# An expert-tile loop on the vector engine that begins at another instruction of the same sequence

## What is computed

```python
logits = xn @ en.T / tau
expert_idx = np.argmax(logits, axis=1)
...
for e in range(E):                      # E = 8 experts
    mask = expert_idx == e
    if not mask.any():
        continue
    h = np.maximum(x[mask] @ w1[e], 0.0)             # 512 -> 1024
    out[mask] = gate_w[mask, None] * (h @ w2[e])     # 1024 -> 512
```

## Time and profile before

| | us |
|---|---|
| median of 3 runs | 1535.5 (1533.52 to 1538.3) |
| the profiled execution's own time | 1540.79 |
| its span, first to last instruction | 1539.0 |
| TensorE busy in the span | 1442.9 (94%) |
| VectorE busy in the span | 920.7 (60%) |

### The profile page before, as it was taken

One profiled execution on the slowest core, in us unless ns is written; L12 is line 12 of the kernel. 1 busy time (PEld: TensorE's weight loads), 2 busy tenths in 40 slices (PEclk: granted clock), 3 DMA queues, 4 the chain that ended last, 5 costly groups with the idle time before them and its releaser, 6 DMA issues.

```text
span 1539.0 us, 27343 instructions
## 1 busy us (share of the span) xinstructions
PE 1442.9 (94%) x8080; PEld 1226.6 (80%) x8081; DVE 920.7 (60%) x1784; ACT 768.3 (50%) x1559; POOL 397.7 (26%) x348
## 2 busy tenths in 40 slices
PE   4799999999999999999999999999999899899996
PEld 3678888888888888888888888877888778678785
DVE  7886677878577878667887766675314123232221
ACT  3666666675657666656666566652323123132220
POOL 3433233334233343324333323231000000000000
PEclk9899999999999999999999999998999999999999
DMA  9532012212001221101121002025312211311110
GB/s 193 148 94 79 1 45 47 64 36 53 9 25 44 47 68 34 37 1 52 42 65 40 22 1 76 1 97 193 116 44 90 94 42 53 131 34 47 41 39 25
DMA packets 139524, 91.18 MB, mean 59 GB/s; under 512 B 118873, under 2 KB 119129, under 8 KB 139233
## 3 DMA queue, kind: packets, MB, share of 16 engines
q1 hardware_dynamic: 132784, 70.12, 17.1%
q0 software_dynamic: 5840, 18.92, 3.3%
q10 hardware_dynamic: 736, 0.29, 0.1%
HBM read 70.39 MB, written 21.28 MB: 60 GB/s over the span
## 4 chain that ended last, share of the span: by engine, by line
PE 56%; DVE 22%; issue 10%; ACT 6%; POOL 3%; DMA 1%; DVEq 1%; ACTq 1%; SPq 0%; POOLq 0%
PE ps L530 17%; PE ps L531 17%; PE ps L532 17%; DVE gs L1003 5%; DVE gs L1000 2%; DVE kfold L1029 2%; ACT gs L804 2%; DVE gs L1008 2%; PE ps L713 2%; DVE k_sb L1035 2%; DVE qrec L1022 1%; POOL g_lo L1397 1%; DVE ps L1001 1%; ACT q_sb L831 1%; PE ps L685 1%
## 5 line engine op out<-in xcount | busy, mean ns | idle before, releaser
L1397 POOL TENSOR_TENSOR g_lo<-gs,g_hi 128x384 fp32r<-128x384 f32 x192 | 205.3, 1069 | 420.2 <-ACT g_hi L809 419.0
L530 PE MATMUL ps<-x_hi,wi_hi 128*128 128x384 f32 x768 | 277.0, 361 | 0.8 <-issue 0.8
L531 PE MATMUL ps<-x_lo,wi_hi 128*128 128x384 f32 x768 | 261.4, 340 | 0.0
L532 PE MATMUL ps<-x_hi,wi_lo 128*128 128x384 f32 x768 | 261.2, 340 | 0.0
L530 PE MATMUL ps<-wo_hi,g_hi 128*128 128x512 f32 x576 | 233.1, 405 | 26.5 <-POOL g_lo L1397 26.2
L531 PE MATMUL ps<-wo_lo,g_hi 128*128 128x512 f32 x576 | 231.0, 401 | 0.0
L532 PE MATMUL ps<-wo_hi,g_lo 128*128 128x512 f32 x576 | 229.6, 399 | 0.0
L799 ACT ACTIVATE usq<-ps 128x384 f32<-128x384 f32 x192 | 93.8, 488 | 250.8 <-PE ps L532 250.8
L920 ACT ACTIVATE hb<-ps 128x512 f32<-128x512 f32 x74 | 44.3, 598 | 330.9 <-PE ps L532 330.9
L1000 DVE SCALAR_TENSOR_TENSOR gs<-gs,ps 128x384 f32<-128x384 f32 x192 | 106.0, 552 | 169.0 <-ACT gs L804 167.5
L1003 DVE TENSOR_TENSOR gs<-gs,usq 128x384 f32<-128x384 f32 x192 | 175.4, 914 | 0.0
(11 more groups left out here) (209 smaller groups left out, 2698.8 us busy)
## 6 DMA issues: line engine op xcount, KB each, us to landing
w_raw<-w SPq DMA_DIRECT2D x10, 2048.0 KB, 9.0
xrow<-scratch SPq DMA_DIRECT2D x37, 257.0 KB, 2.7
q_sb<-q SPq DMA_DIRECT2D x62, 144.0 KB, 3.0
k_sb<-k SPq DMA_DIRECT2D x62, 144.0 KB, 3.1
v_sb<-v SPq DMA_DIRECT2D x60, 144.0 KB, 3.3
in_raw<-w_in SPq DMA_DIRECT2D x8, 512.0 KB, 5.9
out_raw<-w_out SPq DMA_DIRECT2D x8, 512.0 KB, 5.6
scratch<-pad_d SPq DMA_DIRECT2D x8, 257.0 KB, 4.5
```

Of the source, the lines that this page charges most:

```text
L530: mm(out_, a_hi, b_hi, start=first, stop=False)
L531: mm(out_, a_hi, b_lo, start=False, stop=False)
L532: return mm(out_, a_lo, b_hi, start=False, stop=last)
L1397: G.tensor_tensor(g_lo[:, (s - 1) % 3], gs[:, (s - 1) % 2], g_hi[:, (s - 1) % 3].bitcast(F32), ALU.subtract).then_inc(glo_ready, 1)
```

## The change

The body that was `slot` (splits, then scaling) is cut in two. `splits(t)` is all of a tile but the scaling. The loop's turn now begins with `scaled(4i)` and ends with `splits(4i + 4)`; `splits(4)` is written out ahead of the loop and `scaled(32)` behind it. The sequence of vector work that is executed stays the same, instruction for instruction: what moves is the place in it at which the branch back is taken. The other four engines' programs are as before.

```diff
-        def slot(t, j, ahead1, ahead2, stored):
-            with live(dve, t):
-                if ahead1:
-
-                    weights(t, T_SOLE, range(4))
-                h_split(t, j)
-                if ahead2:
-                    with live(dve, t + 2):
-                        t_split(t + 2, (j + 2) % 4)
-                if ahead1:
-                    weights(t, T_NEW, (0, 1))
-                    weights(t, T_SECOND, (2, 3))
-                scaled(t, j, stored)
+        def splits(t, j, ahead1, ahead2):
+
+            if ahead1:
+                weights(t, T_SOLE, range(4))
+            h_split(t, j)
+            if ahead2:
+                with live(dve, t + 2):
+                    t_split(t + 2, (j + 2) % 4)
+            if ahead1:
+                weights(t, T_NEW, (0, 1))
+                weights(t, T_SECOND, (2, 3))
...
-        slot(3, 3, True, True, None)
+        splits(3, 3, True, True)
+        scaled(3, 3, None)
+        splits(4, 0, True, True)
         with dve.Fori(1, LOOPS) as i:
             for j in range(4):
-                slot(i * 4 + j, j, True, True, i * 16)
-        for t in range(4 * LOOPS, TILES):
-            slot(t, t % 4, t + 1 < TILES, t + 2 < TILES, 16 * (t // 4))
+                scaled(i * 4 + j, j, i * 16)
+                splits(i * 4 + (j + 1), (j + 1) % 4, True, True)
+        scaled(4 * LOOPS, 0, 16 * LOOPS)
+        for t in range(4 * LOOPS + 1, TILES):
+            with live(dve, t):
+                splits(t, t % 4, t + 1 < TILES, t + 2 < TILES)
+                scaled(t, t % 4, 16 * (t // 4))
```

## The result

| | before | changed |
|---|---|---|
| median | 1534.5 us (1533.0 to 1538.3, 4 runs) | 1514.3 us (1512.5 to 1516.1, 4 runs) |
| span of the profiled execution | 1539.0 us | 1510.6 us |
| granted clock, mean | 0.981 | 0.988 |

The ratio is 0.9864, with a 95% interval of 0.9842 to 0.9887: 20 us faster, between 17 and 24. The forecast was 1512.1 us, 23.4 us faster.

A forecast was written before the change was run, and what follows sets the result against it. TensorE was taken to bound the kernel, stalled by VectorE's late h_lo at six branches back. Idle 15.6 us plus 7.8 us of slower matmuls make 23.4; 1535.5 - 23.4 = 1512.1 us, range 1508.5 to 1519.

The forecast's parts named there:

- What bounds the kernel: Expert tiles: TensorE, 94% busy, waits 18.3 us for VectorE's h_lo, late behind six branches back; 15.6 us idle there.
- The pauses are the fetch of code: At VectorE's branch back, pauses of 2.87 and 1.94 us were taken for fetching code not on the engine.
- the second question of the prediction: Whether VectorE's pauses go away or are only covered; expected gone, the sum hardly depending on it.
- The three pieces against four: VectorE's old loop body was placed in four 8 KB code pieces, the new one in three, so pauses should go.
- The rival that the stall is not the branch's: Stall belongs to table reading or what follows tile 4i + 3, staying before h_lo; no change, 1535.5 us; chance 0.06.
- The cover and the slack: Moved branch back has 5.4 us of idle cover before osb; osb may then be 4.2 us late at no cost.
- the turn of tile 24: VectorE also writes weights there, so less cover: 0.3 us cost for one pause, 2.2 us idle for both.
- slower: Rival: pause outgrows cover, slack and old loss, above 13.5 us a turn; at 16 us a turn, 1550 us; chance 0.03.
- The size: Gain of 23.4 us: all six stretches holding a branch back fall to 12.50 us, 15.6 idle plus 7.8 slower matmuls.

The follow-up runs named there:

- a_fill71: Changed kernel with 71 never-executed instructions ahead of the loop, so it begins, modulo 128, where the loop of before begins; 1515.7 us, ratio 0.9890.
- a_again10: Changed kernel with the first scaling of each loop turn made 10 times more, so osb comes late; 1561.8 us, ratio 1.0176.
- b_same: Kernel before, unchanged, run once more for a second profile; its six stretches lost 19.6 us.
- b_fill128: Kernel before with 128 never-executed instructions in tile 3's skipped T_SOLE body, ahead of the loop; 1534.0 us, ratio 0.9997.
- a_long128: Changed kernel with 128 never-executed instructions inside the loop, in the skipped T_SOLE body of tiles 4i + 1; 1516.6 us, ratio 0.9886.
- a_again4: Changed kernel with the first scaling of each loop turn made 4 times more; 1518.9 us, ratio 0.9894.

## Why the prediction was right, and where it was off

*What bounds the kernel* held. Of TensorE's 18.3 us of standing still behind `h_lo`, the 15.6 us at the six branch backs came back, and the slower matmuls behind them too; the 2.7 us at the last tile stayed.

*The pauses are the fetch of code* held, and the second question of the prediction, whether they would go or only be covered, came out as expected: they went. The three pieces against four, on which this rested, were bracketed by the kernels with 60, 112 and 128 dead instructions. The rival that the stall is not the branch's falls with the same three: the same work in the same order with the same branches loses 20 us or none by where the code lies. For the price of the branch itself the traces show 0.3 us to code that is there. To code that is not there they show 2.4 to 3.5 us in most turns, and 4.0 to 6.9 us in one turn of five profiles with the VectorE loop in four pieces, each time beside a weight transfer. The prediction says that the fetch shares the transfer queues with the weight loads; the trace has code on a queue of its own (q14, the weights on q1), and the longer pauses beside weight loads are what it shows.

*The cover and the slack* were not needed for the gain, but were true where they were put to the test: 3.4 to 4.5 us of pause in front of `osb` are hidden in five of six turns (a_fill71, where the branch back at 1150.4 us stands 5.5 us ahead of `osb`, for the prediction's 5.4), 4.0 us of lateness are free where the prediction had 4.2, and the turn of tile 24 is the one that pays, 1.4 us of idle time between its 0.3 and 2.2. The page that the prediction weighed, the Trainium skill, "Runtime: NRT & Kernel Launch", section Instruction fetch mechanics, has a jump out of a window of two pages fetch. From it the prediction worked out that a loop longer than one page keeps its pause, and that did not come true: 288 instructions jump back in 0.3 us from their third piece to the first. The rule itself is not refuted by this. Its two pages are 512 instructions, which is four of this trace's pieces; a loop in three pieces lies inside that, and a loop in four, with one more fetched ahead (5 packets a turn), does not. What the trace does not agree with is the page size: this queue moves 8 KB at a time.

The price of the *slower* rival was wrong, though nothing hung on it. The prediction set its break-even at 5.4 + 4.2 + 23.4/6 = 13.5 us of pause, as if the 3.9 us lost in a turn were all idle time. In a_again10 `osb` is 7.85 us late, as a pause of 5.4 + 7.85 = 13.3 us would make it, and the six turns other than that of tile 24 lose 110.7 - 75.0 = 35.7 us, 5.9 each. The break-even is shorter than the prediction had it.

*The size* was the term that was off. The sum took the six stretches of one execution, 23.4 us, and that execution lay 5.3 us above the median of the runs. The loss varies from one execution to the next, by the idle time (15.6 us in the first profile, 13.2 in b_same, 12.3 in b_fill128) and by the clock: tile 12 lost 7.1, 6.6 and 3.9 us in three profiles of this layout, of which 4.4, 4.1 and 3.6 us were idle time, and in the third the granted clock stayed at 1.00. Tile 24 lost 4.5 us when the clock fell and 2.8 us when it did not, for 2.7 and 2.5 us of idle time. The six stretches lose 20.3 us in the mean of the three. The prediction carried the profiled execution's own stalls over to the median without asking whether they explained part of the 5.3 us; about 3 us of it they do, and another 2 us lie ahead of the expert tiles, which began at 1042.3 us in that profile and at 1040.2 and 1040.3 in the two others of this layout. With 20.3 for 23.4, from the later median of 1534.5, the sum gives 1514.2, where 1514.3 was measured. 1512.1 was inside the range all the same.

*What the change was worth as written.* It did two things, and the one that its place in the sequence suggests (to put the branch under idle time) earned nothing here, because the other (57 instructions written out ahead of the loop) had already removed the pause. 60 instructions that do nothing earned the same. Its lasting worth is the insurance, as far as two runs show it (a_fill71, a_long128): with the loop in four pieces it cost 1 to 2 us, not 20.

*Still open:* how many pieces an engine holds was bracketed only from outside (a loop in three pieces brings no packets, one in four brings 5 a turn, which I read as its four and the next; no run separates the two). Why tile 4's stretch is 12.5 us in some profiles and up to 13.0 in others, in both kernels, was not followed up; it is half a microsecond.

## What to carry to other kernels

Where an engine in a hardware loop idles once in each turn with "issue" as the only releaser, look at the sequencer's instructions around the branch back and count the packets of code in a turn: a loop that is a few instructions too long, or that lies a few instructions off, refetches all of its code each turn. Shift it first, which took the pause away here (shortening it should do the same; no run tried it); then put the branch back in front of the wait with the most slack, not in front of the work that the bounding engine waits for. And when a change that reorders code moves the time, compare it with the old order at the new address before crediting the order.

## What the runs showed of the hardware that I had not expected

- Dead code ahead of a loop moves the time by 20 us: with 0, 60, 112 and 128 instructions that are never executed the same kernel takes 1534.5, 1514.7, 1515.7 and 1534.0 us. That fits a period of 128 instructions. If that is one packet of 8 KB, an instruction takes 64 bytes.
- A short stall costs more than its length. In the kernel with ten more scalings 30.4 us of idle time were followed by 15.4 us of slower matmuls: stretches with 3.8 us of idle time had a granted clock of 0.82 to 0.91, part of them at the lower level (1.2 GHz). Behind 0.9 and 1.4 us of idle time the granted clock stayed at 1.00 and the stretch's matmuls took 0.3 us more in all. In between it went either way: it fell to 0.90 behind 2.3 and 2.7 us, and stayed at 1.00 behind 2.5, 2.8 and 3.6 us (tile 24 in b_fill128, the first profile of before, b_same and a_again4; tile 12 in b_fill128).
- What a skip behind a branch back costs goes by how soon it comes. Within 1.0 us of the turn's first instruction it paused for 1.6 to 2.1 us (before, b_same, b_fill128), for 5.0 to 5.4 us at tile 12 of the same three beside a weight transfer, and for 1.3 us in the changed kernel's turn of tile 24 (a_fill71, a_long128). In the other turns of those two it came 1.8 to 3.9 us behind and paused for 0.5 us, even where it jumps over 128 instructions.
